# Pacing SyncE's load queue: each load from chunk 6 on waits for the third load ahead of it

## The reference

```python
# 1. linear attention with decay, H=8 heads of D=64, in blocks
for each block:   out = (q k^T * Dmask) v + (q * lam^(i+1)) state
                  state = lam^block * state + (k * lam^(last-i))^T v
x = out, heads side by side                       # (2, 768, 512)
# 2. channel mix, d_ff = 1024
xk = mu_k * x + (1 - mu_k) * x_prev ;  xr = mu_r * x + (1 - mu_r) * x_prev
x = sigmoid(xr @ w_r) * (relu(xk @ w_k)^2 @ w_v)
# 3. gated mix
gate = sigmoid(causal convolution of x over 5 taps)
out = (gate * (x @ w_val)) @ w_out
```

## Time and profile before

| | us |
|---|---|
| median of 3 runs | 276.83 |
| lowest and highest run | 275.75, 277.29 |
| the profiled execution, its own time | 276.0 |
| its span | 274.2 |
| PE busy in it | 269.9 (98%) |
| DVE, ACT, POOL busy in it | 166.0, 125.4, 23.6 |

### The profile page before, as it was taken

How to read it: one execution, slowest core, us unless ns; L and a number is a source line. 1 busy time by engine, 2 the same in 40 slices (tenths; PEclk the granted TensorE clock), 3 DMA queues, 4 the chain that set the end, 5 groups by cost and what they waited for, 6 DMA issues and landing times.

```text
span 274.2 us, 4270 instructions
## 1 busy us (share of the span) xinstructions
PE 269.9 (98%) x1746; PEld 226.3 (83%) x1746; DVE 166.0 (61%) x258; ACT 125.4 (46%) x223; POOL 23.6 (9%) x25
## 2 busy tenths in 40 slices
PE   8999999999999999999999999999999999999996
PEld 7889977888888888888888888888888888888886
DVE  5866999998581125465885553429969599325000
ACT  2237788977582124365721234748217306412121
POOL 1667750000000000000000000000000000000000
PEclk9999999999999999999999999999999999999999
DMA  7999996000000000000000000530000000310323
GB/s 215 408 410 406 406 407 253 0 0 2 0 0 0 2 0 0 0 2 0 0 0 2 2 0 0 174 134 0 0 0 2 0 0 0 117 38 0 115 82 111
DMA packets 7506, 22.57 MB, mean 82 GB/s; under 512 B 960, under 2 KB 1216, under 8 KB 7488
## 3 DMA queue, kind: packets, MB, share of 16 engines
q1 hardware_dynamic: 7488, 22.31, 21.4%
HBM read 19.16 MB, written 3.15 MB: 81 GB/s over the span
## 4 chain that ended last, share of the span: by engine, by line
PE 96%; DVE 2%; DMA 1%; issue 0%; ACT 0%
PE ps L717 28%; PE ps L719 28%; PE ps L718 28%; PE ps L799 4%; PE ps L733 4%; PE ps L783 2%; PE ps L761 2%; DMA prm<-in_prm 1%; DVE dec L608 1%; DVE pT L508 0%; DVE qdec L589 0%; ACT out_sb L414 0%
## 5 line engine op out<-in xcount | busy, mean ns | idle before, releaser
L717 PE MATMUL ps<-xk_h,wk_h 128*128 128x512 f32 x96 | 37.5, 391 | 0.0
L718 PE MATMUL ps<-xk_l,wk_h 128*128 128x512 f32 x96 | 37.4, 389 | 0.0
L719 PE MATMUL ps<-xk_h,wk_l 128*128 128x512 f32 x96 | 37.4, 389 | 0.0
L717 PE MATMUL ps<-kk_h,wv_h 128*128 128x512 f32 x96 | 37.3, 389 | 0.0
L718 PE MATMUL ps<-kk_l,wv_h 128*128 128x512 f32 x96 | 37.3, 389 | 0.0
L719 PE MATMUL ps<-kk_h,wv_l 128*128 128x512 f32 x96 | 37.3, 389 | 0.0
L571 DVE SCALAR_TENSOR_TENSOR gate<-x,prm,gate 128x512 f32<-128x512 f32 x48 | 32.6, 748 | 0.0
L547 DVE SCALAR_TENSOR_TENSOR kk_f<-ps,ring 128x512 f32<-128x512 f32 x24 | 16.6, 691 | 24.1 <-ACT ring L367 24.1
L384 ACT ACTIVATE gate<-x,prm 128x512 f32<-128x512 f32 x12 | 8.7, 725 | 43.2 <-DVE x L557 43.2
L367 ACT ACTIVATE ring<-ps 128x512 f32<-128x512 f32 x24 | 14.3, 597 | 26.7 <-PE ps L719 26.7
L717 PEld LDWEIGHTS ps<-xk_h,wk_h 128*128 128x128 f32 x96 | 18.0, 188 | 4.0 <-issue 0.3
(11 more groups left out here) (74 smaller groups left out, 487.5 us busy)
## 6 DMA issues: line engine op xcount, KB each, us to landing
qk<-in_qk SPq DMA_DIRECT2D x12, 512.0 KB, 11.3
kv<-in_kv SPq DMA_DIRECT2D x9, 512.0 KB, 12.8
out<-out_sb SPq DMA_DIRECT2D x11, 256.0 KB, 2.0
wk_raw<-in_w_k SPq DMA_DIRECT2D x4, 512.0 KB, 14.2
wv_raw<-in_w_v SPq DMA_DIRECT2D x4, 512.0 KB, 12.5
wr_raw<-in_w_r SPq DMA_DIRECT2D x2, 512.0 KB, 15.0
w_raw<-in_w_val SPq DMA_DIRECT2D x2, 512.0 KB, 4.4
w_raw<-in_w_out SPq DMA_DIRECT2D x2, 512.0 KB, 6.9
```

The costliest lines, as they stand in the source:

```text
L717: nc.tensor.matmul(to, left(0), right(0), start=(i == 0), stop=False)
L718: nc.tensor.matmul(to, left(0), right(1), start=False, stop=False)
L719: done = nc.tensor.matmul(to, left(1), right(0), start=False, stop=(i == last))
```

## The change

From the load of qk6 on, SP waits ahead of a load until the third load ahead of it in its queue has fully landed. So no more than three of these loads are on their way at a time. The order of the loads, their sizes, buffers and semaphores stay as they were, and so do the first loads down to kv5, the waits in `free(n)`, the loads of w_v, and everything on the other engines. The last load that waits in the new way is the second piece of w_r.

```diff
+            def qk_landed(n):
+
+                sp.wait_ge(qk_here[n % IN_BUFS], 16 * (n // IN_BUFS + 1))
+
+            def kv_landed(n):
+
+                sp.wait_ge(kv_here[n % IN_BUFS], 16 * (n // IN_BUFS + 1))
+
...
             load_kv(4)
             load_kv(5)
             for p in range(3, NP - 1):
+                qk_landed(2 * p - 1)
                 load_qk(2 * p)
+                kv_landed(2 * p - 2)
                 load_qk(2 * p + 1)
+                kv_landed(2 * p - 1)
                 load_kv(2 * p)
+                qk_landed(2 * p)
                 load_kv(2 * p + 1)
+            qk_landed(NCH - 3)
             load_qk(NCH - 2)
+            kv_landed(NCH - 4)
             load_qk(NCH - 1)
+            kv_landed(NCH - 3)
             load_weight(wk_raw, w_k, 0, wk_here)
+            qk_landed(NCH - 2)
             load_kv(NCH - 2)
+            qk_landed(NCH - 1)
             load_kv(NCH - 1)
-            for i in range(1, 4):
-                load_weight(wk_raw, w_k, i, wk_here)
-            for i in range(2):
-                load_weight(wr_raw, w_r, i, wr_here)
+            sp.wait_ge(wk_here[0], 16)
+            load_weight(wk_raw, w_k, 1, wk_here)
+            kv_landed(NCH - 2)
+            load_weight(wk_raw, w_k, 2, wk_here)
+            kv_landed(NCH - 1)
+            load_weight(wk_raw, w_k, 3, wk_here)
+            sp.wait_ge(wk_here[1], 16)
+            load_weight(wr_raw, w_r, 0, wr_here)
+            sp.wait_ge(wk_here[2], 16)
+            load_weight(wr_raw, w_r, 1, wr_here)
             sp.wait_ge(att_done, IN_BUFS)
             sp.wait_ge(update_done, updates(IN_BUFS - 1))
             for i in range(4):
```

## The result

| | us |
|---|---|
| before, median (5 runs) | 276.83 |
| after, median (5 runs) | 280.72 |
| after, lowest and highest | 280.37, 282.46 |
| the profiled execution after: own time, span | 280.86, 279.1 |

The changed kernel is slower by a ratio of 1.0159, 95% interval 1.0124 to 1.0194: some 4 us (the two medians lie 3.9 us apart, the two profiled spans 4.9). The forecast was 276.9. The chances had 0.14 on slower, and the range ended at 278.2.

A forecast was written before the change was run, and what follows sets the result against it. PE's work, with loads streaming beside it, was taken as the bound. Between 0 and 0.1 us of late loads was expected; 0.1 was added to the 276.83 us median, giving 276.9 us, range 275.8 to 278.2.

The forecast's parts named there:

- What bounds the kernel: From 8.33 to 40.65 us PE's work and the loads run side by side without gaps; tightest load qk7, 0.5 us early.
- When the next load is asked for: On SP from qk6: a new load reaches the engines within 1.6 us, under 1.9 us of queued work; cost 0.
- The other bound: Paced loads from qk6: each needs 3.9 us after the third ahead lands, as into an empty queue; costs PE 0.1 us.
- The w_v and w_r loads: cost 0: SP issues w_v near 38 us, not 31.83, but it lands about where it did, long before PE needs it; cost 0.
- Rival A: Loads from 19.3 us slow to 1.63 us each with three queued; PE 2.0 us later, 278.8 us; chance 0.13.
- the four w2 loads: Loads of w_val and w_out after 173 us: first takes 3.9 us, the next three 1.63 us each.
- The signs named for it: Scores waiting for qk or update for POOL's decayed k, and under 360 GB/s between 20 and 36 us.
- Rival B: PE's unexplained 0.6 us "issue" stall in attend(8), at L799, goes away with pacing: 276.2 us; chance 0.12.

The follow-up runs named there:

- depth 3: The changed kernel itself: each load from qk6 on waits for the third load ahead of it; ratio 1.0159 to the kernel before.
- depth 4: The changed kernel with each paced load waiting for the fourth load ahead instead of the third; ratio 1.0052 to the kernel before.
- depth 5: The changed kernel with each paced load waiting for the fifth load ahead instead of the third; ratio 0.9998 to the kernel before.
- e12: The kernel before, with the four loads of w_val and w_out issued one at a time, each when the last has landed; ratio 0.9977.
- depth 2: The changed kernel with each paced load waiting for the second load ahead instead of the third; 289.99 us, ratio 1.0494 to the kernel before.
- e16: The changed kernel, with POOL's decayed q of chunk 11 also waiting for DVE's low part of w_k's first piece; ratio 1.0175 to the kernel before.
- e2: The changed kernel with each paced load waiting for the sixth load ahead instead of the third; ratio 1.0011 to the kernel before.
- e10: The kernel before with a single new wait: qk8 waits for the third load ahead, qk7; ratio 1.0047, its traced execution 278.7 us.
- e15: The same kernel as e10, run again: a single wait, at qk8 for qk7, added to the kernel before; ratio 1.0034, its traced execution 276.56 us.

## Why the prediction was wrong

**What bounds the kernel.** Right. Loads and PE run side by side, the slack of each load was read rightly, and PE is late by what the loads are late over it: scores(11), wanted at 33.6, starts at 37.2, when qk11 has landed.

**When the next load is asked for.** This step failed. It said that when qk5 lands, kv4 and kv5 are still queued, 1.9 us of work (2.56 us at later loads), and took the 1.6 us of a small store as the time after which a new load takes part in the stream. So the engines were never to run dry. But a load has landed only when its last part has, and by then the engines have gone on with the next loads. The queue rows from the start to the landing of qk5, before (0 to 17.37) and after (0 to 17.32), settle it:

```profile
q1 hardware_dynamic: 1840, 5.75, 89.0%
q1 hardware_dynamic: 1839, 5.73, 85.1%
```

The loads down to qk5 hold 5.00 MB (nine and a half of 0.524 and the parameters), so 0.75 and 0.73 MB of the 0.79 MB of kv4 and kv5 had already begun: the 1.9 us of queued work were nearly gone when SP asked for qk6. The next 1.85 us of the changed kernel show the engines at 0.58 of their time and 169 GB/s, where they had 1.05 and 414 (last two numbers):

```profile
17.33:19.18 1.85, 1.82 (x36) 1.63 (x40) 1.13 (x4) 1.07 (x4) 1.63 (x2) 1.00 0.58 169
```

By the same 0.75 MB, an estimate: depth 3 leaves 0.3 MB or 0.7 us of work at 408 GB/s in place of 2.56, depth 4 leaves 2.0 us and depth 5 leaves 3.3. The 0.7 us don't cover the 1 us after which a lone load's data flow. That depth 4 still loses rate with 2.0 us left says that such a mean isn't the whole story: some engines must have less left than others. How much of the 0.75 MB is engines that run apart and how much is the time from the last byte to the semaphore, these rows don't tell. Between 20 and 40 us the queue rows show the engines idle for a tenth of the time and each packet 20% slower.

**The other bound.** This was the number that should have saved the range, and it was no bound. It took the 3.9 us of a load in an empty queue as the most that a paced load can need. A lone load does take 3.5 to 4.2 us (e12). But the time isn't hidden under the loads queued ahead; a good part of it comes on top: 4.6 us at depth 2, 5.6 at depth 3, where I had 3.9 for both. The period follows, 1.76 us where I had 1.30. (Its sum also let kv6 land 0.7 us behind qk7, less than the 1.28 us of a load; that changes nothing here.)

**The w_v and w_r loads: cost 0.** Wrong as a reading, without a cost of its own in the changed kernel. SP was to issue w_v near 38 and issues it at 45.55. At 1.76 us a load w_r and w_v are many microseconds late, and ACT and DVE, which do their lists in order, bring xr so late that PE has no slack left at 69 us; in e16 it waits 0.7 us there and at depth 2 3.2 us. I had followed the lists only up to w_k.

**Rival A.** The right mechanism with the right place and the right threshold: 1.43 us a load was its price point, and depth 4, at 1.46, loses 0.5%, depth 5, at 1.32, nothing. It was given 0.13. I set the four w2 loads aside as first touches after a long rest; e12 shows that the first touch isn't what makes a lone load take its time. Its price was 2.0 us against a measured 4: the real period is 1.76 and not 1.63, by which its own sum gives 19.3 + 17.6 = 36.9 and 3.3 us, and on the way DVE's list met POOL's. The signs named for it came true, 2.8 us of waits for paced qk loads and 302 GB/s between 20 and 36 us. Both figures that it and the other bound take from the Trainium skill's page "DMA: Bandwidth & Descriptors" (sections "Bandwidth" and "Anatomy of one DMA") are given there for DMAs issued from GpSimd, and SP issues these. For a lone 512 KB load that page's formula is an estimate of 3.2 us; the four here took 3.5 to 4.2.

**Rival B.** Its stall did go away in the changed kernel, and came back in e2 at no loss of speed. Whether the shallow queue took it away or PE's lateness did isn't shown; its gain of 0.6 us came at no depth.

**The range.** Its lower end was argued as rival B less half of the runs' spread, which is 275.5 and not 275.8. Its upper end left out rival A's full size knowingly, and the measured time lies beyond even that.

**Left open.** Why packets get slower when less is queued, and which part of the engines runs empty at a single wait (e10, e15): the trace doesn't name the engine of a packet. That e10's 2.56 us of queued work were hardly more than 0.7 us follows from the 0.75 MB above.

## What to carry to other kernels

A transfer's start-up isn't free just because other transfers are queued ahead of it: measure issue-to-landing at the depth you mean to run, and divide by the depth. Here five 512 KB loads in flight, about 2.5 MB, cost no time and give 94% of the rate; six give all of it, three 74%. And when a load is reported as landed, don't count all that was issued behind it as still to do: look how much of it has been moved already. When the one row that speaks against a forecast comes from "special" circumstances, that is a reason to widen the range, not to drop the row. And where engines work through lists in order, follow a late load through each list to the next place where PE waits: there can be a second bound right behind the first.

## What the runs showed of the hardware

The rate of a load stream grew steadily with its depth, 253, 301, 350, 384 and 408 GB/s for two to six loads of 512 KB. When a load of the deep stream is reported as landed, 0.75 MB behind it has begun.

After the 2.13 us stop of PE in e10 the granted clock fell for some microseconds. Rows of e10: stretch, length, PE, PEld (weight loads), DVE, ACT, POOL, PEclk, DMA share, GB/s:

```profile
26.00:30.00 4.00, 2.56 (x56) 2.41 (x53) 3.94 (x6) 2.17 (x6) 1.59 (x2) 1.00 1.01 393
30.00:32.00 2.00, 1.30 (x20) 0.88 (x19) 0.77 (x2) 1.39 (x3) 0.71 (x1) 0.83 1.02 379
32.00:36.00 4.00, 4.00 (x66) 3.97 (x64) 4.00 (x5) 1.71 (x5) 3.26 (x3) 0.66 0.99 366
```

1.00 is 2.4 GHz; 0.83 and 0.66 are stretches partly at 1.2 GHz. attend of two chunks took 3.27 us there and 1.97 elsewhere:

```profile
32.03 3.27 PE L802 MATMUL ps<-pT,kv 128*64 128x128 f32 x32
...
38.14 1.97 PE L802 MATMUL ps<-pT,kv 128*64 128x128 f32 x32
```

So 1.3 us was paid on top of the stop. In the changed kernel, whose waits are 1.2 us at most, and at depth 2, whose waits before 50 us are 1.65 us at most, the clock stayed at 1.00.
